# More filler products on TensorE between routing and the first expert of an attention, mixture and gated convolution kernel

## The reference

```python
x = attention(q, k, v, s).transpose(0, 2, 1, 3).reshape(B, S, H * D)      # 4 x 576 x 512
logits = x @ w_gate                                                       # 8 experts
local_gate = sigmoid(x @ w_local)
e = argmax(logits[b, s]) if s == 0 or local_gate[b, s] < 0.5 else prev_e  # one expert a token
out[b, s] = softmax(logits[b, s])[e] * (relu(x[b, s] @ w1[e]) @ w2[e])    # 512 -> 1024 -> 512
...
h = relu(out @ w_in)                                                      # 512 -> 1024
gate = sigmoid(conv3(h, conv_w))
result = (h * gate) @ w_out
```

## Time and profile before

| | us |
|---|---|
| median of 3 runs | 755.36 |
| the three runs | 758.05, 754.62, 755.36 |
| the profiled execution | 752.84 |
| its span in the profile | 751.1 |
| mean granted clock of TensorE | 0.995 |

### The profile page before, as it was taken

The page is one execution under the profiler, slowest core; times in us unless marked ns, Lnnn a source line. Parts: engine busy times, 40 slices in busy tenths (PEclk is TensorE's granted clock), DMA queues, the critical chain, the costliest instruction groups (busy, mean ns, idle before and its releaser), DMA issues.

```text
span 751.1 us, 15066 instructions
## 1 busy us (share of the span) xinstructions
PE 737.3 (98%) x4945; PEld 625.1 (83%) x4945; DVE 437.3 (58%) x1041; ACT 319.6 (43%) x628; POOL 328.5 (44%) x442
## 2 busy tenths in 40 slices
PE   8999999999889999999999999999999999999998
PEld 5787888878777888888888888888899889889986
DVE  4778788788777545454545444444489555636510
ACT  3777788777530013111111311100388344535620
POOL 7658788878415468644444775400421100000000
PEclk9999999999999999999999999999999999999999
DMA  8898988774154765434334443300421110000011
GB/s 179 206 239 224 222 214 224 205 190 105 33 170 141 252 197 201 158 125 160 120 149 136 144 148 127 122 29 15 136 75 27 52 36 15 28 29 15 29 43 56
DMA packets 99848, 93.39 MB, mean 124 GB/s; under 512 B 62124, under 2 KB 71620, under 8 KB 99780
## 3 DMA queue, kind: packets, MB, share of 16 engines
q1 hardware_dynamic: 80340, 46.53, 23.3%
q10 hardware_dynamic: 15968, 34.67, 13.5%
q0 software_dynamic: 3472, 11.28, 5.2%
HBM read 76.13 MB, written 16.33 MB: 123 GB/s over the span
## 4 chain that ended last, share of the span: by engine, by line
PE 69%; DVE 1%; DMA 1%; ACT 0%; issue 0%; DVEq 0%; ACTq 0%; POOLq 0%
PE wide_bank L1258 18%; PE row_bank L1273 18%; PE wide_bank L1508 14%; PE row_bank L1546 13%; PE wide_bank L1294 3%; PE bank L1224 1%; PE bank L1477 1%; DMA x_slots<-x_rows,token_of 1%; PE bank L1497 0%; ACT apart L1113 0%; PE row_bank L1497 0%; ACT row_is L1116 0%; PE bank L1488 0%; PE row_bank L1488 0%; DVE h_tr L1362 0%
## 5 line engine op out<-in xcount | busy, mean ns | idle before, releaser
L891 POOL TENSOR_TENSOR ring<-raw_w,ring 128x2048 fp32r<-128x2048 f32 x28 | 128.6, 4616 | 89.4 <-ACT ring L881 89.4
L1258 PE MATMUL wide_bank<-ring,xs_tr 128*128 x600 | 143.3, 394 | 1.2 <-DVE xs_tr L1334 0.8
L1273 PE MATMUL row_bank<-ring,h_tr 128*128 x600 | 143.8, 394 | 0.3 <-DVE h_tr L1362 0.3
L881 ACT ACTIVATE ring<-raw_w 128x2048 fp32r<-128x2048 f32 x30 | 55.8, 1908 | 200.2 <-DMA raw_w<-in_moe_w_dram 171.0
L1273 PEld LDWEIGHTS row_bank<-ring,h_tr 128*128 128x128 f32 x600 | 110.8, 188 | 23.3 <-issue 0.7
L1258 PEld LDWEIGHTS wide_bank<-ring,xs_tr 128*128 128x128 f32 x600 | 110.7, 188 | 23.4 <-issue 1.6
L1508 PE MATMUL wide_bank<-x_tr,ring 128*128 128x288 f32 x768 | 107.7, 297 | 0.0
L1508 PEld LDWEIGHTS wide_bank<-x_tr,ring 128*128 128x128 f32 x768 | 103.2, 188 | 0.9
L1546 PE MATMUL row_bank<-ring,g_tr 128*128 128x512 f32 x432 | 100.1, 389 | 0.0
L1546 PEld LDWEIGHTS row_bank<-ring,g_tr 128*128 128x128 f32 x432 | 80.4, 188 | 16.1
L678 ACT ACTIVATE prob<-score,row_min 128x128 f32<-128x128 f32 (+2 forms) x144 | 83.2, 579 | 18.1 <-DVE row_min L541 15.9
(11 more groups left out here) (234 smaller groups left out, 994.3 us busy)
## 6 DMA issues: line engine op xcount, KB each, us to landing
raw_w<-in_moe_w_dram ACTq DMA_DIRECT2D x12, 2048.0 KB, 10.0
ncum_row<-cum_rows SPq DMA_DIRECT2D x15, 512.0 KB, 5.4
y_sorted<-y_sb SPq DMA_DIRECT2D x26, 256.0 KB, 2.9
raw_w<-in_moe_w_dram SPq DMA_DIRECT2D x12, 512.0 KB, 3.9
ncum_tail<-cum_rows SPq DMA_DIRECT2D x32, 144.0 KB, 4.5
out_dram<-out_sb ACTq DMA_DIRECT2D x18, 256.0 KB, 2.0
v_nat<-in_v_dram SPq DMA_DIRECT2D x32, 128.0 KB, 2.9
q_nat<-in_q_dram SPq DMA_DIRECT2D x30, 128.0 KB, 4.0
```

The source lines that it names most:

```text
L881: nc.scalar.activation(high, whole, ACT.Copy).then_inc(high_ready, 1)
L891: nc.gpsimd.tensor_tensor(low, whole, high.bitcast(F32), ALU.subtract).then_inc(low_ready, 1)
L1258: last = nc.tensor.matmul(h_bank[:, half, :], xs_tr[:, a, kb, :], ring[:, bass.ds(n, 1), b, at:at + FH].rearrange("p a c -> p (a c)"), sta ...
L1273: last = nc.tensor.matmul(y_bank[:, :], h_tr[:, a, kb, :], ring[:, bass.ds(n, 1), 2 + b, kb * D:(kb + 1) * D].rearrange("p a c -> p (a c)" ...
```

## The change

It adds fillers at four places in TensorE's queue. Amid the first table's products, one filler behind t = 1, 4, 7, 10, 13 and 16 (t % 3 == 1 and not the last). Behind the first table, six in place of five. Behind the turn of the convolution's weights, nine in place of five. Behind the turn of the first slot's x, two where there were none. All write wide_bank[1][:, 0, :]. No wait and no other instruction changes.

```diff
                 last = nc.tensor.matmul((bank[1], row_bank[1])[part][:, 0:slots.stop - slots.start], row_is[:, t, :], slot_token[:, t, slots],
                                         start=t == 0, stop=t == T - 1)
+
+                if part == 0 and t % 3 == 1 and t < T - 1:
+                    keep_running(nc, wide_bank[1][:, 0, :], identity, 1)
             last.then_inc(tokens_summed, 1)
             if part == 0:
-                keep_running(nc, wide_bank[1][:, 0, :], identity, 5)
+                keep_running(nc, wide_bank[1][:, 0, :], identity, 6)
         pe.wait_ge(conv_loaded, 16)
         nc.tensor.transpose(row_bank[0][:, 0:K * KF], conv_nat[:, :], identity[0:K * KF, 0:K * KF]).then_inc(conv_turned, 1)
-        keep_running(nc, wide_bank[1][:, 0, :], identity, 5)
+        keep_running(nc, wide_bank[1][:, 0, :], identity, 9)
...
         n = weights_of(0, 0)
         turn_first_x()
+        keep_running(nc, wide_bank[1][:, 0, :], identity, 2)
         hidden(0, (0,), n)
```

## The result

Over 16 runs each, beside each other, the changed kernel has a median of **753.63 us** (752.87 to 755.06) and the kernel before 755.8 (754.13 to 759.43). The ratio is 0.9973, with a 95% interval of 0.9961 to 0.9985: 0.27% faster, a gain of 2.2 us where I had forecast a loss of 0.3. The time lies inside the predicted range, near its lower end, and inside the 0.5% that I had called "same"; the direction was wrong, and the interval excludes no change. That the range holds the time is no merit of the sum: with the spread alone it would have ended at 754.0, and only the 0.6 us added for rival B bring in 753.63.

The account below looks back on a forecast made before the run. TensorE, busy 98% of the span, was taken as the bound, so fillers could act only around routing. Median 755.36 plus 0.3 us for the fillers amid the table, all else nothing, gave 755.7 us; range 753.4 to 757.8.

Parts of the forecast that it names:

- the sum: Whole kernel: 0.3 us of delay from the table fillers, nothing from the other parts, added to the median 755.36.
- the spread: Range of the forecast: half the 3.4 us spread of three runs, 1.7 us on either side, giving 754.0 to 757.4.
- rival B: First expert products: a clock fall there, in executions without one at 219.6, is spared; 1.6 us saved, 754.1; chance 0.18.
- Step (5): Clock around routing: the fall at 219.65 to 223.00 goes, but nobody waits there, so gain on the path 0.
- Step (1): Six fillers amid the first table: its last products 0.35 us late, +0.3 us at the end, bounds 0 and +0.55.
- the sign: Check on the table fillers' delay: ScalarE's last row_is to token_of grows from 0.32 us to about 0.65.
- rival A: Gather of slot 0: its landing is set by the weight load, so it swallows the table's delay; 755.4; chance 0.2.
- step (3): Nine fillers for five behind the conv weights: no cost, 0.9 us of cover; the value loads aren't held either.
- Steps (2) and (3): Sixth filler behind the first table, nine behind the conv weights: no cost, with 1.4 and 0.9 us of cover.
- Step (4): Two fillers behind the turn of x: 0.45 us in a 0.85 us gap, no cost, 0.4 us of cover left.
- Rival C: Ahead of the turn of x: half-clock fillers end 0.5 us past x's arrival, so slower, 756.5; chance 0.12.
- Rival D: First table: the fillers don't hold the clock, the fall stays at about 219.6; 755.7 to 755.8; within the forecast's 0.45.

Follow-up runs that it names:

- e1: The kernel before, unchanged: median 755.56 us, ratio 1.0004; its profile has twelve first expert products at 4.60 us.
- e16: Single profiled execution of the kernel before, unchanged: span 754.5 us, 537.8 from row to end, twelve products 4.60.
- e2: The kernel before plus only the six fillers amid the first table: median 755.47 us, ratio 1.0.
- e7: The changed kernel with five in place of nine fillers behind the conv weights: median 754.64 us, ratio 0.9992 to the kernel before.
- e15: Single profiled execution of the kernel before, unchanged: span 752.1 us, 536.1 from row to end, twelve products 3.01.
- e14: Single profiled execution of the kernel before, unchanged: span 755.0 us, 538.5 from row to end, twelve products 5.33.
- e5: The kernel before without any of the ten fillers behind the two tables: median 756.33 us, ratio 1.0009.
- e9: The kernel before with only nine in place of five fillers behind the conv weights: median 754.83 us, ratio 0.9996.
- e3: The kernel before with only six for five fillers behind the first table and nine for five behind the conv weights: median 753.49 us, ratio 0.9977.
- e8: The changed kernel without the six fillers amid the first table: median 753.82 us, ratio 0.9987 to the kernel before.
- e12: The changed kernel with slot 0's two values as constants and without the fillers amid the table: median 753.57 us, ratio 0.9996 to the kernel before.
- e17: Single profiled execution of the changed kernel without the fillers amid the first table: span 751.7 us, 535.8 from row to end.
- e4: The kernel before plus only the two fillers behind the turn of the first x: median 755.18 us, ratio 0.9998.
- e10: The changed kernel with slot 0's two values as constants, value loads only ahead of slot 1: median 753.5 us, ratio 0.9986 to the kernel before.

## Why the prediction was wrong

**Step (5), the gain on the path, was set to 0 from one execution.** This is the step that failed. Five profiled executions of the kernel before show four with a fall on the path, three of them on the products. The text had the mechanism as rival B, with its price of 1.6 us (measured: 4.60 - 3.03 = 1.57 in the products of e1 and e16), and gave it a chance of 0.18. B's condition was too narrow as well. It wanted executions in which the fall at 219.6 is missing, so that the fillers end early. The edited kernels e2 and e7 show that order, but e1 and e16 have the harmless fall and a second one on the products, in e15 one fall lasts from the fillers through the turn, and e14's begins at 222.2 with no account. The profile had given a warning that I explained away: the median of the runs stood 2.5 us above the profiled execution. I wrote that nothing in the change alters what lies between them, and held against B that one fall is too small for it. A fall can be 6.8 or 10.2 us long as well (e2, e5 and e14), on the turn too, and then costs 2.6 to 2.7 us from row to end.

**Step (1)** was right in size: 0.35 us worked out, 0.32 measured, and 0.64 us from ScalarE's last row_is to token_of, where the sign was about 0.65. What became of it was half right. The gather was 0.31 us shorter, as rival A had it, but that it was so for starting later isn't shown: in the profiles without fillers amid the table whose chain shows it, it took 3.52 to 3.98 us. And the turn of x didn't profit, for the value loads behind slot_ready had moved along with VectorE. My reading of the value loads in step (3), from the start of the first load alone, overlooked that the second one ends at 224.1, beside the landing. The turn came 0.33 us later behind `row`, and the end 0.3.

**Steps (2) and (3)**: the second table starts at 220.36, the nine fillers end at 223.38, and the turn waits for neither; no cost, as said. **Step (4)**: four passes in the gap, 0.40 us of cover left, as said; but no gain of their own either. **Rival C** did not come about in any profile of the changed kernel; in e9, with the fall at 219.3, the fillers end just as the turn begins, at no cost. The Trainium skill, TensorE: Matmul & The Clock Gate, section LDWEIGHTS (loading the stationary operand), gives a weight load's time as its columns over 1.2 GHz, with no term for the clock's level. The trace disagrees: the fillers' loads lasted 186 to 192 ns in the changed kernel, at 1.00, and up to 333 ns within the fall of e9; the 18 passes took 2.27 us and 3.14. **Rival D** didn't happen: the changed kernel's profiles have no fall at 219.6. Nor have those of e3, e8, e12 and e17, so the fillers amid the table aren't needed for that.

**The sum** from this: by the profiles, 1.4 us less from `row` to the end, which holds the 0.3 us that the fillers amid the table cost; so the falls on the path that are gone would be worth some 1.7 us. The times have 2.2 and 1.1 us.

What stays open: how many executions of e9 and e7 have the fall on the path; whether the fillers amid the table ever prevent one there (the four profiles without them, with six and nine behind the tables, have none); what the sixth filler behind the table does; what starts a fall such as e14's; and the size of the gain, 2.2 us in one group and 1.1, not resolved, in another. Of the versions with nine fillers behind the conv weights, only the change in its first comparison and e3 are faster beyond their intervals.

## What to carry to other kernels

A profile is one draw: where the granted clock or a race decides, look at several executions before an effect is priced at nothing, and take a profiled time well below the median of the runs as a sign that the profile missed something. Fillers paid here where they stood ahead of long work on TensorE's path, in time that it would have idled through (e7 against the changed kernel); fillers at other places, amid the table (e2) or behind the turn (e4), gave nothing that the times show. The fillers between products that others wait for cost 0.32 us, at the last of these products.

## What the runs showed of the hardware that I had not expected

An execution with the turn of x at 224.59 had the clock fall at 226.38, and one with it at 224.28, of the same kernel, did not the earlier trace rows. From `row` on, falls lasted 3.4 us in five profiles (two each in e1 and e16), 6.8 in e2, e4 and e15, and 10.2 in e5 and e14. At half clock the four transposes of the turn took 1.09 us in place of 0.63, and the twelve products of 512 columns up to 5.44 in place of 3.0. And the two value loads on TensorE's queue took from 222.7 to 224.1 us with their checks, the first 0.8 us; without them the turn began 0.43 us sooner behind `row` (e10).
